# Second half of a weight product as three passes on high and low parts, with w1 and w2 brought in halves

## The reference

```python
# attention with a recurrent state, for 32 heads (4 batches x 8), 768 steps, 40 dims
m_new = max(f_gate[t] + m, i_gate[t])
C = exp(f_gate[t] + m - m_new) * C + exp(i_gate[t] - m_new) * outer(v[t], k[t])
n = exp(f_gate[t] + m - m_new) * n + exp(i_gate[t] - m_new) * k[t]
y[t] = sigmoid(o_gate[t]) * (C @ q[t]) / max(abs(n @ q[t]), 1)
# x: y with the heads side by side, 3072 tokens x 320
x1 = ((x @ w1) * (x @ w2)) @ w3 @ w_out          # w1, w2 320x1024, w3 1024x1024, w_out 1024x320
out = max(x1 @ v1, x1 @ v2, x1 @ v3) @ v_out     # v1, v2, v3 320x768, v_out 768x320
```

## Time and profile before

| what | value |
|---|---|
| median of 3 runs | 688.51 us (688.37 to 691.78) |
| the profiled execution | 688.5 us |
| its span, first to last instruction | 686.7 us |
| TensorE busy | 679.0 us, 99% of the span |
| VectorE busy | 396.2 us, 58% |
| ScalarE busy | 284.6 us, 41% |
| GpSimd busy | 120.6 us, 18% |
| granted TensorE clock, mean | 0.999 |
| prologue, up to the first product of `body(0)` | 61.48 us |

### The profile page before, as it was taken

The page is one execution under the profiler, slowest core; times in us unless marked ns, Lnnn a source line. Parts: engine busy times, 40 slices in busy tenths (PEclk is TensorE's granted clock), DMA queues, the critical chain, the costliest instruction groups (busy, mean ns, idle before and its releaser), DMA issues.

```text
span 686.7 us, 10623 instructions
## 1 busy us (share of the span) xinstructions
PE 679.0 (99%) x3456; PEld 564.3 (82%) x3456; DVE 396.2 (58%) x855; ACT 284.6 (41%) x600; POOL 120.6 (18%) x155
## 2 busy tenths in 40 slices
PE   9999999999999999999999999999999999999997
PEld 6787888788888888888888888888888888888785
DVE  7577888754676733676743576753567743322423
ACT  1556765433655312655322555422545422222211
POOL 4423333020233200133300043200023100000000
PEclk9999999999999999999999999999999999999999
DMA  7999586240556310454410355510164100100001
GB/s 237 320 267 221 165 204 156 58 126 10 142 125 139 95 39 0 118 143 122 122 38 0 89 132 142 134 38 0 52 145 121 47 1 1 38 1 0 1 1 38
DMA packets 39077, 65.70 MB, mean 96 GB/s; under 512 B 4180, under 2 KB 21908, under 8 KB 39044
## 3 DMA queue, kind: packets, MB, share of 16 engines
q1 hardware_dynamic: 38532, 64.57, 35.1%
q10 hardware_dynamic: 512, 0.70, 0.3%
HBM read 58.00 MB, written 4.03 MB: 90 GB/s over the span
## 4 chain that ended last, share of the span: by engine, by line
PE 95%; DVE 2%; DMA 1%; ACT 1%; issue 0%; SPq 0%; DVEq 0%; POOL 0%; ACTq 0%
PE ring L519 55%; PE acc L519 24%; PE ybank L519 11%; PE sbank L519 4%; PE tbank L519 1%; DMA qk_s<-in_qkT 1%; PE tbank L626 1%; DVE hid L1089 0%; DVE gm L1070 0%; ACT gm L773 0%; DMA vn_s<-in_vn 0%; DVE x1T L1189 0%; DVE ab_rem L978 0%; ACT c_part L773 0%; ACT left L773 0%
## 5 line engine op out<-in xcount | busy, mean ns | idle before, releaser
L519 PE MATMUL ring<-x1T,mx_hi 128*128 128x512 f32 x432 | 152.8, 394 | 0.7 <-ACT x1T L773 0.5
L519 PE MATMUL ring<-xT,ab_hi 128*128 128x512 f32 x384 | 136.7, 397 | 0.0
L773 ACT ACTIVATE gm<-hid 128x512 fp32r<-128x512 f32 x84 | 53.1, 632 | 166.3 <-DVE hid L1089 129.7
L481 POOL TENSOR_TENSOR decay_s<-decay_s,causal 128x512 f32<-128x512 f32 x41 | 54.1, 1319 | 381.9 <-DMA qk_s<-in_qkT 375.2
L519 PE MATMUL acc<-gm,wp 128*128 128x512 f32 x384 | 96.9, 395 | 0.0
L519 PEld LDWEIGHTS ring<-x1T,mx_hi 128*128 128x128 f32 x432 | 81.1, 188 | 18.7 <-issue 0.9
L773 ACT ACTIVATE left<-ring 128x512 f32<-128x512 f32 x84 | 49.9, 594 | 92.2 <-PE ring L519 92.2
L519 PEld LDWEIGHTS acc<-gm,wp 128*128 128x128 f32 x384 | 71.7, 188 | 16.0
L1070 DVE TENSOR_TENSOR gm<-hid,gm 128x512 fp32r<-128x512 f32 x84 | 58.2, 692 | 46.0 <-ACT gm L773 46.0
L519 PEld LDWEIGHTS ring<-xT,ab_hi 128*128 128x128 f32 x384 | 72.2, 188 | 14.8 <-DVE hid L1077 0.3
L519 PE MATMUL ring<-x1T,mx_lo 128*128 128x512 f32 x216 | 84.2, 390 | 0.0
(11 more groups left out here) (150 smaller groups left out, 919.4 us busy)
## 6 DMA issues: line engine op xcount, KB each, us to landing
qk_s<-in_qkT SPq DMA_DIRECT2D x40, 480.0 KB
decay_s<-phi_d SPq DMA_DIRECT2D x41, 256.0 KB, 4.4
kg_s<-in_kg SPq DMA_DIRECT2D x40, 160.0 KB, 5.6
vn_s<-in_vn SPq DMA_DIRECT2D x48, 84.0 KB, 2.1
w_raw<-in_w3T SPq DMA_DIRECT2D x7, 512.0 KB, 6.0
out_y<-stage SPq DMA_DIRECT2D x11, 256.0 KB, 2.2
c_st<-c_part SPq DMA_DIRECT2D x24, 105.0 KB
stage<-in_wmax SPq DMA_DIRECT2D x6, 384.0 KB, 4.3
```

The lines of the kernel that those rows point to most:

```text
L481: pool.tensor_tensor(d4, d4, causal[:].unsqueeze(1).broadcast_to([P, HQ, L]), ALU.add).then_inc(s["masked"], 1)
L519: return pe.matmul(o, l, r, start=start, stop=stop)
L773: return act.activation(o, i, ACT.Copy)
```

## The change

The first half of the result is formed as before. The second half (`split_step`) is formed in three fp32r passes. For that `w_out` and pieces 4 to 7 of `w3` are split: high parts on ScalarE (`w1_high`, `w3_split_high`), low parts on VectorE (`w1_low`, `w3_split_low`). The high part of `w3` overwrites pieces 0 to 3 of the raw `w3` when their products are done, the low parts overwrite the raw values, and the high part of `w_out` lies in the still empty half of `wp`. The columns of w1 and w2 are laid out in halves, so that the first three `ab` pieces hold what tiles 0 to 3 of the first block need; TensorE enters `body(0)` after three pieces and waits for all six ahead of tile 4. In the prologue three `ab` pieces are split in place of six, at its end; all other pieces move back, and the loads with them. The first product step moves ahead of the gates' transpose.

```diff
+        over_w3 = ExitStack()
+        w3_split = sb("w3_split", [P, W3_PIECES, W3_TILES, FF1 // 2], F32R, over_w3)
+        w1o_lo = sb("w1o_lo", [P, AB_TILES, MODEL], F32R, over_w3)
+        over_w3.close()
...
-        beside1 = [[], [N_AB, N_AB + 1], [N_AB + 2], [N_AB + 3], [N_AB + 4], [N_AB + 5], [N_AB + 6], []]
-        beside2 = [[N_AB + 7], [N_AB + 8], [N_AB + 9], [N_AB + 10], [], []]
+        early_loads = [[], [], [], [], [], [0], [1, 2], [3]]
+        early_hi = [[], [], [], [], [], [], [0], [1]]
+        beside1 = [[3], [4, 5], [6], [7], [8], [9], [10], []]
+        beside2 = [[11, 12], [13], [14, 15], [16], [], []]
+        loads_beside = [[], [4, 5], [6], [7, 8], [9], [10], [11], [12]]
+        loads_behind = [13, 14, 15, 16]
```

SyncE in the prologue:

```diff
-                if k + 1 < W3_PIECES:
-                    load_w3(k + 1)
+                for t in {2: [3], 3: [4], 4: [5, 6], 5: [7]}.get(k, []):
+                    load_w3(t)
...
-                load_piece(k - 1)
+                for n in early_loads[k]:
+                    load_piece(n)
```

TensorE, the second half of the product and the entry to the first block:

```diff
+            def split_step(t, j, tiles=range(4)):
+                n, k = t - W3_PIECES // 2, (t - W3_PIECES // 2) * W3_TILES + j
...
+                pe.wait_ge(s["w1_hi"], n + 1)
+                pe.wait_ge(s["w3_hi"], n + 1)
                 for i in tiles:
+                    if k == 0 and i >= 2:
                         pe.wait_ge(s["wp_ok"], i - 1)
+                    mm(bank_of(i), part(w3_high(t), i), w1o_hi[:, k, :], k == 0, False)
+                pe.wait_ge(s["w1_lo"], n + 1)
+                for i in tiles:
+                    mm(bank_of(i), part(w3_high(t), i), w1o_lo[:, k, :], False, False)
+                pe.wait_ge(s["w3_lo"], n + 1)
+                for i in tiles:
+                    last = mm(bank_of(i), part(w3_low(t), i), w1o_hi[:, k, :], False, k == AB_TILES - 1)
...
-                    pe.wait_ge(s["part_done"], N_AB)
+                    pe.wait_ge(s["part_done"], N_FIRST)
                 for i in range(AB_TILES):
+                    if isinstance(c, int) and c == 0 and i == AB_TILES // 2:
+                        pe.wait_ge(s["part_done"], N_AB)
```

ScalarE in the prologue, behind `first_gate(k + 1)`:

```diff
+                if k == 1:
+                    w1_high(0)
+                    w1_high(1)
+                if k == 2:
+                    w1_high(2)
+                    w1_high(3)
                 if k == 3:
+                    w3_split_high(4)
                     product_hi(0)
-                if k >= 2:
-                    piece_hi(k - 2)
+                if k in (4, 5, 6):
+                    w3_split_high(k + 1)
+                for n in early_hi[k]:
+                    piece_hi(n)
             first_out(QUADS - 1)
+            piece_hi(N_FIRST - 1)
             x_hi(0, 0)
```

VectorE in the prologue:

```diff
                     weigh(0, k)
-                    if k >= 3:
-                        piece_lo(k - 3)
+                    if k == 3:
+                        w3_split_low(4)
+                    if k == 4:
+                        w1_low(3)
+                    if k in (5, 6, 7):
+                        w3_split_low(k)
+                    if k == 7:
+                        piece_lo(0)
                     normaliser(0, k - 1)
                     gate_out(0, k - 1)
+                    if k == 2:
+                        w1_low(0)
+                        w1_low(1)
+                    if k == 3:
+                        w1_low(2)
-            piece_lo(N_AB - 1)
+            piece_lo(1)
             normaliser(0, QUADS - 1)
             gate_out(0, QUADS - 1)
+            piece_lo(2)
             x_lo(0, 0)
             c_lo(0)
```

## The result

The changed kernel takes 697.94 us (median of 4 runs, 695.96 to 698.96) against 688.71 for the kernel before (4 runs, 688.37 to 691.78). The ratio is 1.0126, with a 95% interval of 1.0112 to 1.0140: slower by 1.3%, and outside the range that was predicted. The profiled execution took 698.13 us, 9.6 more than that of before, so its trace holds the whole loss.

The account below looks back on a forecast made before the run. The prediction took TensorE, busy 679.0 of 686.7 us, as the bound, with VectorE tight at the entry to `body(0)`. It summed +1.28 (late loads) and +0.90 (`left` copy) to +2.2 on 688.5: 690.7 us, range 687.8 to 692.6.

Parts of the forecast that it names:

- The loads behind: Entry to chunk 1: `qk_s` issued at about 57.0, landing 64.4, `k_lo` done at 67.0; scores and tile 1 move +1.28 us.
- A second price of 0: Second block: `stack_state(1)` goes later by about one tile's work; `x_hi` of chunk 1, two tiles on, priced at 0.
- A third: Prologue: the first product step ahead of the gates' transpose only exchanges work on a busy TensorE, priced at 0.
- The waits beside quads 5 and 6: Prologue: TensorE stands about 0.95 us for `w3` low parts behind `weigh`; quad 5 costs +0.2, quad 6 +0.6.
- The `wo` copy in front of the `left` copy: Second block, ScalarE: a `wo` copy ahead of `c_hi(1)` delays tile 1's `left` copy, +0.90 us.
- The step of k=7: Prologue, TensorE: quad 7's product step starts at 52.54, only 0.06 us earlier than before.
- The last `x_lo`: Entry to `body(0)`, VectorE: done at 64.07 where it was 63.33; TensorE waits, +0.74 us, later replaced by +1.28.
- The wait for `k_st` that was to show: Sign near 66 us: TensorE waits about a microsecond for `k_st`, GpSimd's mask waiting for `qk_s` until past 63.
- The saving arrives: Rival, chance 0.07: VectorE delivers low parts in time and the left copy isn't last; -3.2, 685.3 us.
- Only the entry is cheap: Rival, chance 0.20: `qk_s` lands early, masks miss `q_lo`; +0.7 there, left copy 0 to 0.9; 688.9 to 690.1 us.
- The loads are late: Rival, chance 0.20: `qk_s` lands 9.1 us after issue, at 66.1; +3.0, with 0.9 it is 692.4 us.
- VectorE later still: Rival, chance 0.08: a pass of 0.169 adds 0.6, a mask on `c_lo` 0.9; 691.3 to 692.2 us.

Follow-up runs that it names:

- the last experiment: Changed kernel with loads and pieces reordered, plus `w3` high parts ahead of ScalarE's gate and two `w_out` low parts behind the bank-freeing copies: 686.94 us, ratio 0.997 to before.

## Why the prediction was wrong

**The step that failed** is the one under "The loads behind" that followed chunk 1's first loads only: `qk_s`, `kg_s`, values. It never went on to `stack_state(0)`, which stands in the same queue behind two more pieces, and set no price on `c_st`; nor had its sum any term for a slower clock behind a wait. The runs showed there 2.59 us of wait (2.6 in the trace with pieces earlier, 3.8 with the plain product) and 3.5 us of half clock behind it: 6.1 of the 9.6 us. Small pieces 4 and 5 take the wait away, other work through the wait takes the half clock away. That the state has pieces ahead of it was not new; how close they stand was. In the kernel before, the last piece's issues and the state's behind them read:

```profile
57.18 1.56 SPq L314 DMA_DIRECT2D stage<-in_wmax  x2
62.15 5.66 SPq L366 DMA_DIRECT2D c_st<-c_first  x6
```

There that piece and the one before it, 768 KB, were issued by 58.74, over 3 us ahead of the state, and no wait for `c_st` shows; now 1 MB ends at 63.15, and the state starts at 63.93.

**A second price of 0** was `stack_state(1)`: the prediction saw that its load goes later and left it to the upper end. It cost 0.94 us, by the same pattern (`x_hi(1, 0)` waits for the state, and the `left` copy is behind it).

**A third**, the first product step, was priced at 0. Alone it costs nothing that can be told (0.9995). In the profile of the full change it cost about 0.4, since `w1o_raw` came 5.71 us after issue. What made that landing later than in the other trace isn't shown.

**Rightly predicted.** A pass takes 0.146 us (0.150 predicted; twelve in 1.76). The waits beside quads 5 and 6 were 1.07 and 0.82 (0.95), and there was none beside 7. The `wo` copy in front of the `left` copy cost 0.9 (0.90). `qk_s` was issued at 57.99 and the mask began at 64.65 (57.0 and 64.4). This agreement is in part luck: the issue came 1.0 us later than predicted, and the load took 6.7 us to land in place of 7.4.

**Off in size.** The step of k=7 came at 53.60 (52.54 predicted): 0.4 from the first step, 0.2 from k=4, whose gain of 0.5 was 0.26 by the timelines, and 0.3 from k=5, where from the step's start to the low part it was 2.48 us (41.77 to 44.25) in place of 2.15; 0.1 is from k=6. The last `x_lo` was done at 65.10 (64.07), and the scores came at +1.63 (+1.28). The wait for `k_st` that was to show didn't: TensorE had stood 1.11 us for `x_lo` first, and `k_lo` was done at 67.35, just as the passes ahead of the scores ended.

**The rivals.** The saving arrives: not in this kernel, and only in part in the last experiment, 1.9 us of 3.2. Only the entry is cheap: no. The loads are late: the nearest in kind, a landing behind a piece, but it had the wrong load, `qk_s`, and no half clock. VectorE later still: by 1 us, but not by its reasons: no mask lay on `c_lo`, and a pass was cheaper. `q_lo`, from two SBUF tiles, took 1.12 us where the mask ran until 65.94, against 0.68 for `x_lo`. The Trainium skill ("SBUF — State Buffer", Who interferes with whom) has such a pair exclude each other where the GpSimd instruction reads SBUF, as the mask does; the trace agrees.

The sum therefore reads: predicted +2.2; measured 1.63 (to the scores) + 2.59 + 3.5 + 0.9 + 0.94 = 9.6 us.

## What to carry to other kernels

When loads move, follow the whole queue to the last transfer that anything waits for, and above all to one that is needed soon and stands behind big ones that are not: the state, six transfers of 105 KB, waited here for 1 MB of weights. A standstill of the matrix engine of a microsecond or more can cost more than twice its length, for the clock may halve behind it. And before a faster product is judged, look at what its inputs stand behind on their engines: here two edits of order, on ScalarE and VectorE, took the time from 0.5% above the kernel before to 0.3% below it.

## What was not expected of the hardware

- **The clock.** After a standstill of 2.59 us the granted clock was 0.50 from 78 to 82 us, with TensorE busy for the whole of it; after one of 2.28 us it was 0.64 on the mean of 40 to 44. With TensorE kept busy it was 1.00 throughout. The fall need not come at once: when the changed kernel was traced once more, after a standstill of 3.2 us, it was still 1.00 from 76 to 78 us, then 0.74 and 0.50; and with the low parts first, where TensorE stood for 5.98 us, it was already 0.61 from 76 to 78 us, while TensorE still stood. The length of one standstill doesn't decide it alone: 1.7 us in the last experiment left the clock at 1.00, while the 1.04 us with the state's transfer ahead were followed by 0.57 on the mean of 84 to 88 us. What parts these two isn't shown. The Trainium skill ("TensorE: Matmul & The Clock Gate", HAM oscillation — how this bites in real kernels) describes this as an effect of waits for transfers, and advises to arrange the work so that they don't fall between products; the traces agree.
- **Landing times.** The last `c_st` transfer took 8.03 to 9.02 us from issue to landing in five traces with pieces 4 and 5 ahead of it, and 12.59 in a sixth; piece 5 in its place took 8.34. The Trainium skill ("DMA: Bandwidth & Descriptors", Queues, rings and completion order) says that each DMA engine takes the descriptors of one ring in order, and that the increment of the semaphore lands only behind that engine's earlier writes; that the wait goes when pieces 4 and 5 shrink agrees. Why it was 12.59 in one run isn't shown.
